# Column-half key sums, a state of own blocks only, and 64-row state products in a linear-attention, gating, Fourier and MLP kernel

## The chip, the cores and the metric

The kernel runs on one core of a Trainium2 chip. The metric is the time of one execution in microseconds (us), as the device measures it; lower is better. The engines are PE (TensorE, matrix products; its weight loads are recorded apart as PEld), DVE (VectorE), ACT (ScalarE), POOL (GpSimd) and SP (here the queue that issues the loads). They run side by side and wait for each other by semaphores.

## The reference, cut to what matters

Three stages run over 4 batch entries of 768 tokens. The first is a linear attention with decay, of 8 heads with 48 features each:

```
for t in range(S):
    state = alpha[:, :, t, :, None] * state + np.einsum('bhd,bhe->bhde', k[:, :, t], v[:, :, t])
    y[:, :, t] = np.einsum('bhd,bhde->bhe', q[:, :, t], state)
```

Its output (384 features a token) goes through a causal depthwise convolution of 5 taps whose sigmoid gates `x @ w_val`, then through `w_out`. The last stage adds the real part of a 2-D Fourier transform, normalises each token, and adds `max(un @ w_ch1, 0) @ w_ch2` with 1536 hidden features.

## The kernel before

**Attention by chunks.** The 768 tokens of a batch entry are taken in 6 chunks (`c` = 0 to 5) of 128. The 8 heads stand in 4 pairs (`p`, `NP` = 4): the even head of a pair (`e` = 0) has its 48 key features on partitions 0 to 47, the odd one (`e` = 1) on 64 to 111. For each chunk:

- `load`, `inv`, `scale` (DVE): scans that form the running decays, then the decayed keys `kd` and queries `qd`.
- `scores`: PE transposes `kd` into the PSUM bank `sums` (L881, 4 transposes) and forms the scores of each head from 48 rows, even heads into the bank `evens`, odd heads into `odds` (L886, 8 matmuls). ACT copies the transposes to `kdT` (L580). Not needed after chunk 5, so there the transposes, the copy and the next two items are left out.
- `sum` (PE, L895): the keys-times-values sum of the chunk, one matmul per pair, 128 stationary columns (both heads' keys) by 112 moving columns of `v_in` (both heads' values). Of the products, those of one head's keys with the other head's values are not needed.
- `state` (DVE, L757 and L761): per head half (64 partitions by 4x48) old state plus new sum, times the decay at the chunk's end. The tile `state` holds 96 columns per pair; the columns of the other head are zero, set once at the start (L703), so that a product over all 128 rows sees one head only.
- `mask` (DVE, L742): both score banks, masked, to `scores`. 
- `y` (PE, `y_of`): output features on partitions, 32 at a time. All outputs go to the bank `evens`, whose blocks 0 and 1 hold the first 32 features (`DA`) of the 8 heads and block 2 the last 16 (`DB`) of each. The part from the state, for c > 0, has 8 matmuls for the first 32 features (L911) and 4 for the last 16 of both heads of a pair (L914), all of 128 rows by 32 stationary columns and 128 moving columns. The part from the scores has 8 (L919) and 8 (L924).
- ACT copies the three blocks to `xT` (L586).

**Order.** Every engine walks the same hand-written list `SCHEDULE`. `prologue()` has the chunks of batch entry 0, with little other PE work among them (`wd` L971, `tapj` L965). `front(b)` has the middle stages of entry b, and for b = 1 and 2 also chunk 0 of the next entry. `mlp(b)` has the MLP of entry b in slots: one `h` (L854, 9 matmuls) and one `down` (L939, 6 matmuls) each; ACT writes `h_hi` (L628) and DVE `h_lo` (L836) between them. The tables `FIRST` and `LATER` put the chunks of entry b + 1 into the slots: `scores` of a chunk two or more slots ahead of its `sum`, `y` and `state`, which stand together. So of the 24 chunks 6 lie in the prologue, 16 in MLP slots (chunk 0 of entry 1, chunks 1 to 5 of entries 1 to 3) and 2 in the fronts. `sum` runs 20 times, the state part of `y` 20 times.

**Waits.** `scores_of` waits for `s_xc` (the bank copied to `xT`) and `s_st` (the state updated, `sums` free); `chunk_sum` for `s_kdc` (`kdT` copied); `y_of` for `s_mask` and `s_st`.

## Time and profile before

| | us |
|---|---|
| median of 3 runs | 596.6 |
| lowest and highest | 596.46, 596.72 |
| the profiled execution | 598.3 |
| its span, first to last instruction | 596.6 |
| PE busy | 581.7 (98%) |
| PE weight loads busy | 553.2 (93%) |
| DVE busy | 393.9 (66%) |
| ACT busy | 198.1 (33%) |

The span of the profiled execution equals the median of the timed runs; 1.7 us of its own 598.3 lie outside the span. In the profile an fp32 matmul appears as two records, so the 4 matmuls of L895 are "x8". Records of PE overlap, so the pace is read from the starts, not from the durations.

### The profile page before, as it was taken

How to read it: one execution, taken by the hardware profiler on the slowest of the kernel's cores; microseconds unless marked ns; L12 is line 12 of the kernel's file. 1: busy time of each engine (PE TensorE's matmuls, PEld its weight loads, DVE VectorE, ACT ScalarE, POOL GpSimd, SP SyncE). 2: the span in 40 equal slices, each digit the busy share in tenths (PEclk: the TensorE clock that was granted, in tenths of full speed). 3: DMA queues.
4: the chain of work that ended last, by engine and by line, in shares of the span. 5: the costliest groups of instructions: out<-in, count | busy, mean ns of one | idle time of the engine just before them, and what ended most of it. 6: DMA issues, size and time to landing. Idle time of an engine off the chain costs nothing.

```text
span 596.6 us, 12364 instructions
## 1 busy us (share of the span) xinstructions
PE 581.7 (98%) x5181; PEld 553.2 (93%) x5181; DVE 393.9 (66%) x835; ACT 198.1 (33%) x437; POOL 14.0 (2%) x31
## 2 busy tenths in 40 slices
PE   7999999999999999999999999999999999999996
PEld 6788999999999999999999999999999999999996
DVE  7579987978948674886947467687855573442221
ACT  5343445424243143324143134222433234222210
POOL 0000000000000000000000000000000000000000
PEclk8999999999999999999999999999999999999999
DMA  7667001232222002033202002033100000000000
GB/s 270 218 220 332 1 18 53 69 113 70 76 73 70 26 3 68 20 120 96 69 11 86 28 2 69 1 89 96 52 1 28 1 27 1 1 2 27 3 25 26
DMA packets 16857, 38.23 MB, mean 64 GB/s; under 512 B 2337, under 2 KB 5410, under 8 KB 16546
## 3 DMA queue, kind: packets, MB, share of 16 engines
q1 hardware_dynamic: 14976, 32.71, 16.5%
q0 software_dynamic: 1536, 4.72, 2.2%
q8 instruction: 41, 0.67, 0.5%
q14 instruction: 14, 0.11, 0.1%
q10 hardware_dynamic: 290, 0.01, 0.0%
HBM read 32.71 MB, written 4.72 MB: 63 GB/s over the span
## 4 chain that ended last, share of the span: by engine, by line
PE 91%; DVE 3%; ACT 2%; issue 2%; DMA 1%; POOL 0%; ACTq 0%; DVEq 0%
PE bank L854 47%; PE bank L939 24%; PE evens L886 4%; PE sums L895 3%; PE bank L965 2%; PE evens L911 2%; PE evens L919 2%; PE evens L924 2%; PE bank L1028 1%; PE bank L1002 1%; PE sums L881 1%; PE bank L971 1%; DVE unT_lo L635 1%; ACT diag L545 1%; PE evens L914 1%
## 5 line engine op out<-in xcount | busy, mean ns | idle before, releaser
L836 DVE SCALAR_TENSOR_TENSOR h_lo<-bank,h_hi 128x256 fp32r<-128x256 f32 x144 | 60.5, 421 | 116.7 <-ACT h_hi L628 113.6
L854 PE MATMUL bank<-unT_hi,w_hi 128*128 128x256 f32 x432 | 125.4, 290 | 2.3 <-DVE unT_lo L635 2.2
L854 PE MATMUL bank<-unT_lo,w_hi 128*128 128x256 f32 x432 | 122.0, 282 | 0.0
L854 PE MATMUL bank<-unT_hi,w_lo 128*128 128x256 f32 x432 | 121.6, 281 | 0.0
L628 ACT ACTIVATE h_hi<-bank 128x256 fp32r<-128x256 f32 x144 | 54.9, 381 | 185.6 <-PE bank L854 185.6
L939 PE MATMUL bank<-w_hi,h_hi 128*128 128x384 f32 x288 | 99.3, 345 | 0.0
L939 PE MATMUL bank<-w_lo,h_hi 128*128 128x384 f32 x288 | 97.7, 339 | 0.0
L939 PE MATMUL bank<-w_hi,h_lo 128*128 128x384 f32 x288 | 97.2, 338 | 0.0
L854 PEld LDWEIGHTS bank<-unT_hi,w_hi 128*128 128x128 f32 x432 | 81.2, 188 | 8.5 <-DVE unT_lo L635 4.5
L854 PEld LDWEIGHTS bank<-unT_hi,w_lo 128*128 128x128 f32 x432 | 81.6, 189 | 0.0
L854 PEld LDWEIGHTS bank<-unT_lo,w_hi 128*128 128x128 f32 x432 | 81.4, 189 | 0.0
L939 PEld LDWEIGHTS bank<-w_hi,h_hi 128*128 128x128 f32 x288 | 54.1, 188 | 2.5 <-issue 2.5
L939 PEld LDWEIGHTS bank<-w_lo,h_hi 128*128 128x128 f32 x288 | 54.1, 188 | 0.0
L939 PEld LDWEIGHTS bank<-w_hi,h_lo 128*128 128x128 f32 x288 | 54.1, 188 | 0.0
L771 DVE SCALAR_TENSOR_TENSOR gate<-xT,wconv,gate 128x384 f32<-128x384 f32 x72 | 42.3, 611 | 0.4
L729 DVE TENSOR_TENSOR_SCAN kd<-a_in,ends 128x516 f32<-128x516 f32 x24 | 29.6, 1233 | 0.8
L720 DVE TENSOR_TENSOR_SCAN lam<-a_in,starts 128x516 f32<-128x516 f32 x24 | 29.4, 1224 | 0.8 <-DMA a_in<-in_alpha_dram 0.8
L586 ACT ACTIVATE xT<-evens 128x384 f32<-128x384 f32 x24 | 11.8, 492 | 49.7 <-PE evens L924 49.7
L886 PE MATMUL odds<-qd,kd 48*128 48x128 f32 x192 | 27.7, 285 | 0.0
L886 PE MATMUL evens<-qd,kd 48*128 48x128 f32 x192 | 27.7, 285 | 0.0
L886 PEld LDWEIGHTS evens<-qd,kd 48*128 48x128 f32 x192 | 23.1, 187 | 4.3 <-issue 4.3
L508 POOL DMA_DIRECT2D out_dram<-u x24 | 13.0, 547 | 576.0 <-DVE u L842 576.0
(159 smaller groups left out, 1102.6 us busy)
## 6 DMA issues: line engine op xcount, KB each, us to landing
a_in<-in_alpha_dram SPq DMA_DIRECT2D x24, 258.5 KB, 2.7
q_in<-in_q_dram SPq DMA_DIRECT2D x24, 256.0 KB, 2.8
k_in<-in_k_dram SPq DMA_DIRECT2D x24, 256.0 KB, 3.2
v_in<-in_v_dram SPq DMA_DIRECT2D x24, 224.0 KB, 3.4
w_raw<-in_w_dram SPq DMA_DIRECT2D x2, 2304.0 KB, 11.5
out_dram<-u POOLq DMA_DIRECT2D x24, 192.0 KB, 2.3
dftd<-in_dft_d_dram SPq DMA_DIRECT2D x1, 582.0 KB, 5.8
woutT<-in_w_out_t_dram SPq DMA_DIRECT2D x1, 576.0 KB, 6.8
```

The lines of the kernel that those rows point to most:

```text
L508: pool.dma_start(out[b, t], u[:, slot(t), :]).then_inc(s_out, 16)
L628: act.activation(h_hi[:, f % HBUF, :], ps[:, 0:GW], ACT.Relu).then_inc(s_hi, 1)
L720: dve.tensor_tensor_scan(lam_[:, :, :].rearrange("d p t -> d (p t)"), a_t[:, 0:NP * CW], starts[:, :, :].rearrange("d p t -> d (p t)"), 0. ...
L729: dve.tensor_tensor_scan(kd_[:, :, :].rearrange("d p t -> d (p t)")[:, ::-1], a_t[:, NP * CW:0:-1], ends[:, NP * CW:0:-1], 0.0, ALU.mult, ...
L771: dve.scalar_tensor_tensor(acc, xT[:, m, t + a * HALF:t + (a + 1) * HALF], wconv[:, m, t:t + 1], acc, ALU.mult, ALU.add).then_inc(s_tap, 1)
L836: dve.scalar_tensor_tensor(h_lo[:, f % HBUF, :], ps[:, 0:GW], 0.0, h_hi[:, f % HBUF, :].bitcast(F32), ALU.max, ALU.subtract).then_inc(s_re ...
L854: last = pe.matmul(ps, l, r, start=(i == 0), stop=(i == len(mms) - 1))
L886: last = pe.matmul(ps[:, p, :], kd_[rows, p, 1:CW], qd_[rows, p, :], start=True, stop=True)
L895: last = pe.matmul(sums[:, p, 0:VW], kdT[:, p, :], v_in[:, c % 2, p, :], start=True, stop=True)
L911: pe.matmul(y[rows, h // 4, :], st[:, h // 2, first:first + DA], qd_[:, h // 2, :], start=(h < 4), stop=False, skip_group_check=True)
L919: pe.matmul(y[rows, h // 4, :], v_[:, h // 2, first:first + DA], scores[:, h % 2, h // 2, :], start=(c == 0 and h < 4), stop=True, skip_gr ...
L939: last = pe.matmul(ps, l[:, f % HBUF, rows], r, start=(f == 0 and x == 0), stop=(f == NF - 1 and x == 2))
```

## The change

- The key sum is 8 matmuls instead of 4: for each pair one per head, 64 stationary columns of `kdT` by that head's 48 columns of `v_in`. The even head's result goes to partitions 0 to 63 of `sums`, the odd head's to 64 to 127, both in columns 0 to 47.
- `state` has 48 columns per pair and no zero blocks, so DVE updates both heads of all pairs in one instruction over 128 partitions, two instructions per chunk instead of four (one instead of two in chunk 0).
- The first 32 features of `y` from the state are 8 matmuls of 64 rows by 32 stationary columns; even heads go to `evens`, odd heads to block 0 of `odds`. The scores part for the first 32 features follows (even heads to `evens`, odd heads to `odds`).
- The last 16 features keep their 128-row products. For these a new tile `tails` holds them with zero blocks. ACT fills it with two copies per chunk (c > 0), placed at `scores`, ahead of the copy to `kdT`; PE waits for the new semaphore `s_tail` between the two groups of state products.
- ACT's copy to `xT` is two instructions, one from each bank. The feature order on the host follows.

```diff
-        state = sb("state", [128, 2, NP, 2 * DH])
+        state = sb("state", [128, 2, NP, DH])
+        tails = sb("tails", [128, 2, NP, 2 * DB])
@@ ACT
-                elif kind == "scores" and a < NCH - 1:
+                elif kind == "scores":
+                    n = b * NCH + a
+                    if a > 0:
+
+                        act.wait_ge(s_st, updates(n - 1))
+                        wait_for(act, s_y, n - 1)
+                        for e, cols in ((0, slice(DA, DH)), (1, slice(0, DB))):
+                            rows = slice(64 * e, 64 * e + 64)
+                            last = act.activation(tails[rows, (a + 1) % 2, :, e * DB:(e + 1) * DB],
+                                                  state[rows, (a + 1) % 2, :, cols], ACT.Copy)
+                        last.then_inc(s_tail, 1)
+                    if a == NCH - 1:
+                        continue
                     act.wait_ge(s_kdT, updates(b * NCH + a))
@@
-                    act.activation(xT[:, :, PAD + a * CH:PAD + (a + 1) * CH], evens[:, 0:K, :],
-                                   ACT.Copy).then_inc(s_xc, 1)
+                    here = slice(PAD + a * CH, PAD + (a + 1) * CH)
+                    act.activation(xT[:, 0:K - 1, here], evens[:, 0:K - 1, :], ACT.Copy)
+                    act.activation(xT[:, K - 1, here], odds[:, 0, :], ACT.Copy).then_inc(s_xc, 1)
@@ DVE
+                    new = sums[:, :, 0:DH]
+                    if c > 0:
+                        dve.tensor_tensor(state_new[:, :, :], new, state[:, (c + 1) % 2], ALU.add).then_inc(s_stn, 1)
+                        dve.wait_ge(s_stn, b * (NCH - 2) + c)
+                        new = state_new[:, :, :]
+                    dve.tensor_tensor(state[:, c % 2], new, fin[:, c % 2, :].unsqueeze(2).broadcast_to([128, NP, DH]),
+                                      ALU.mult).then_inc(s_st, 1)
@@ PE
-                    last = pe.matmul(sums[:, p, 0:VW], kdT[:, p, :], v_in[:, c % 2, p, :], start=True, stop=True)
+                    for e in range(2):
+                        rows = slice(64 * e, 64 * e + 64)
+                        last = pe.matmul(sums[rows, p, 0:DH], kdT[:, p, rows], v_in[:, c % 2, p, e * 64:e * 64 + DH],
+                                         start=True, stop=True)
@@
-                    for h in range(H):
-                        first = h % 2 * (2 * DH - DA)
-                        rows = slice(32 * (h % 4), 32 * (h % 4) + 32)
-                        pe.matmul(y[rows, h // 4, :], st[:, h // 2, first:first + DA], qd_[:, h // 2, :],
-                                  start=(h < 4), stop=False, skip_group_check=True)
                     for p in range(NP):
-                        pe.matmul(y[32 * p:32 * p + 32, 2, :], st[:, p, DA:DA + 2 * DB], qd_[:, p, :],
+                        for e, y in enumerate((evens, odds)):
+                            rows = slice(64 * e, 64 * e + 64)
+                            pe.matmul(y[32 * p:32 * p + 32, 0, :], st[rows, p, e * DB:e * DB + DA], qd_[rows, p, :],
+                                      start=True, stop=False, skip_group_check=True)
+                    pe.wait_ge(s_tail, updates(n - 1))
+                    for p in range(NP):
+                        pe.matmul(evens[32 * p:32 * p + 32, 1, :], tl[:, p, :], qd_[:, p, :],
                                   start=False, stop=False, skip_group_check=True)
```

PE's list, at chunk 1 of batch entry 1 in an MLP slot, before (L854 is `h`, L939 `down`; sizes are stationary by moving columns):

```order
L854 MATMUL bank<-unT_hi,w_lo 128x256
L895 MATMUL sums<-v_in,kdT 128x112 [waits kd_copied,v_loaded_odd]
L895 MATMUL sums<-v_in,kdT 128x112 x3
L911 MATMUL evens<-qd,state 32x128 [waits state_updated,scores_masked]
L911 MATMUL evens<-qd,state 32x128 x7
L914 MATMUL evens<-qd,state 32x128 x4
L919 MATMUL evens<-scores,v_in 32x128 x8
L924 MATMUL evens<-scores,v_in 32x128 x4
L924 MATMUL evens<-scores,v_in 16x128 x4
L939 MATMUL bank<-w_hi,h_hi 128x384 [waits bank_read_vector]
```

The same place after (L861 is `h`, L950 `down`):

```order
L861 MATMUL bank<-unT_hi,w_lo 128x256
L904 MATMUL sums<-v_in,kdT 64x48 [waits kd_copied,v_loaded_odd]
L904 MATMUL sums<-v_in,kdT 64x48 x7
L921 MATMUL evens<-qd,state 32x128 [waits state_updated,scores_masked]
L921 MATMUL odds<-qd,state 32x128
...
L925 MATMUL evens<-qd,tails 32x128 [waits state_tails_copied]
L925 MATMUL evens<-qd,tails 32x128 x3
L930 MATMUL evens<-scores,v_in 32x128 x4
L930 MATMUL odds<-scores,v_in 32x128 x4
L935 MATMUL evens<-scores,v_in 32x128 x4
L935 MATMUL evens<-scores,v_in 16x128 x4
L950 MATMUL bank<-w_hi,h_hi 128x384 [waits bank_read_vector]
```

Nothing moves against `h` and `down`; the sum has twice as many matmuls of narrower shape, the state part as many as before (8 and 4) with the 8 alternating between the banks, and a wait stands ahead of the last 4.

ACT's list in the prologue, around the copy to `kdT` of chunk 2, before:

```order
L553 ACTIVATE wd_hi<-bank 128x388 [waits unit_done]
L559 ACT_TABLE_LOAD
L559 ACTIVATE gate<-bank 128x2x128 [waits unit_done]
L556 ACTIVATE wd_lo<-bank 128x388 [waits unit_done]
L580 ACTIVATE kdT<-sums 128x512 [waits chunk_summed,kd_transposed]
```

And after:

```order
L555 ACTIVATE wd_hi<-bank 128x388 [waits unit_done]
L561 ACT_TABLE_LOAD
L561 ACTIVATE gate<-bank 128x2x128 [waits unit_done]
L558 ACTIVATE wd_lo<-bank 128x388 [waits unit_done]
L587 ACTIVATE tails<-state 64x4x16 [waits y_ready,state_updated]
L587 ACTIVATE tails<-state 64x4x16
L594 ACTIVATE kdT<-sums 128x512 [waits chunk_summed,kd_transposed]
```

The two copies stand ahead of the copy to `kdT` and of all that ACT does later.

## Rows read from the trace of the kernel before

**Rows 1.** The page: busy time and share of the span by engine.
```profile
PE 581.7 (98%) x5181; PEld 553.2 (93%) x5181; DVE 393.9 (66%) x835; ACT 198.1 (33%) x437; POOL 14.0 (2%) x31
```

**Rows 2.** The page: the chain that ended last, share by engine.
```profile
PE 91%; DVE 3%; ACT 2%; issue 2%; DMA 1%; POOL 0%; ACTq 0%; DVEq 0%
```

**Rows 3.** Timeline of PE, chunk 1 of entry 1 (start, length, engine, line, operands, records).
```profile
117.75 0.28 PE L854 MATMUL bank<-unT_hi,w_lo 128*128 128x256 f32 x1
117.87 1.04 PE L895 MATMUL sums<-v_in,kdT 128*128 128x112 f32 x8
118.84 0.64 PE L911 MATMUL evens<-qd,state 128*32 128x128 f32 x16
119.30 0.40 PE L914 MATMUL evens<-qd,state 128*32 128x128 f32 x8
119.52 0.62 PE L919 MATMUL evens<-scores,v_in 128*32 128x128 f32 x16
119.95 0.62 PE L924 MATMUL evens<-scores,v_in 128*32 128x128 f32 x16
120.50 0.44 PE L939 MATMUL bank<-w_hi,h_hi 128*128 128x384 f32 x1
```

**Rows 4.** Timeline of PE, the scores of a chunk between `down` and `h`.
```profile
163.60 0.34 PE L939 MATMUL bank<-w_lo,h_hi 128*128 128x384 f32 x1
163.78 0.34 PE L939 MATMUL bank<-w_hi,h_lo 128*128 128x384 f32 x1
164.05 0.37 PE L886 MATMUL evens<-qd,kd 48*128 48x128 f32 x1
164.05 0.37 PE L886 MATMUL odds<-qd,kd 48*128 48x128 f32 x1
164.26 0.27 PE L886 MATMUL evens<-qd,kd 48*128 48x128 f32 x1
...
164.94 0.27 PE L886 MATMUL odds<-qd,kd 48*128 48x128 f32 x1
165.14 0.39 PE L854 MATMUL bank<-unT_hi,w_hi 128*128 128x256 f32 x1
```

**Rows 5.** Timeline of PE, the sum of chunk 0 in `front(1)`.
```profile
214.62 1.15 PE L895 MATMUL sums<-v_in,kdT 128*128 128x112 f32 x8
215.53 0.34 PE L854 MATMUL bank<-wd_hi,sum_hi 128*128 128x194 f32 x1
```

**Rows 6.** Timeline of PE, chunk 0 of the prologue.
```profile
10.54 2.02 PE L895 MATMUL sums<-v_in,kdT 128*128 128x112 f32 x8 [0.79 <-ACT kdT L580]
12.49 1.08 PE L919 MATMUL evens<-scores,v_in 128*32 128x128 f32 x16
14.14 0.59 PE L971 MATMUL bank<-dftd,woutT 128*128 128x388 f32 x1
```

**Rows 7.** Windows: busy time by engine; the third number from the right is the granted clock.
```profile
10.50:13.60 3.10, 3.06 (x32) 2.81 (x36) 2.94 (x7) 0.00 (x0) 0.00 (x0) 0.50 0.83 321
13.60:14.20 0.60, 0.60 (x17) 0.35 (x9) 0.60 (x2) 0.00 (x0) 0.00 (x0) 0.79 0.00 0
```

**Rows 8.** Timeline of all engines in the prologue, chunks 3 and 4.
```profile
40.04 0.72 DVE L757 TENSOR_TENSOR state_new<-sums,state 64x192 f32<-64x192 f32 x2
40.79 0.72 DVE L761 TENSOR_TENSOR state<-state_new,fin 64x192 f32<-64x192 f32 x2
...
44.55 0.27 PE L886 MATMUL odds<-qd,kd 48*128 48x128 f32 x1
...
45.65 0.69 DVE L742 TENSOR_TENSOR scores<-evens,mask 128x512 f32<-128x512 f32 x1
```

**Rows 9.** Groups by line and form: busy us, mean ns; idle us before, its end.
```profile
L911 PE MATMUL evens<-qd,state 128*32 128x128 f32 x320 | 12.9, 279 | 2.0 <-DVE scores L742 2.0
L628 ACT ACTIVATE h_hi<-bank 128x256 fp32r<-128x256 f32 x144 | 54.9, 381 | 185.6 <-PE bank L854 185.6
L586 ACT ACTIVATE xT<-evens 128x384 f32<-128x384 f32 x24 | 11.8, 492 | 49.7 <-PE evens L924 49.7
```

More of the change, by code:

```diff
@@ L421, in build @@
         s_st = sem("state_updated")
+        s_tail = sem("state_tails_copied")
         s_xc = sem("x_copied")
@@ L702, in _ @@
             dve.memset(mask[:, :], 1.0).then_inc(s_sets, 1)
-            dve.memset(state[:, :, :, :], 0.0).then_inc(s_sets, 1)
+            dve.memset(tails[:, :, :, :], 0.0).then_inc(s_sets, 1)
             dve.memset(xT[:, :, 0:PAD], 0.0).then_inc(s_sets, 1)
@@ L747, in _ @@
                     wait_for(dve, s_y, n)
-                    parts = []
-                    for e in range(2):
-                        rows = slice(64 * e, 64 * e + 64)
-                        mine = slice(e * DH, (e + 1) * DH)
-                        parts.append((state[rows, (c + 1) % 2, :, mine], state[rows, c % 2, :, mine],
-                                      sums[rows, :, e * (VW - DH):e * (VW - DH) + DH], state_new[rows, :, :],
-                                      fin[rows, c % 2, :].unsqueeze(2).broadcast_to([64, NP, DH])))
-                    for old, st, new_ps, new, end in parts:
-                        if c > 0:
-                            dve.tensor_tensor(new, new_ps, old, ALU.add).then_inc(s_stn, 1)
-                    for e, (old, st, new_ps, new, end) in enumerate(parts):
-                        if c > 0:
-                            dve.wait_ge(s_stn, 2 * (b * (NCH - 2) + c - 1) + e + 1)
-                        last = dve.tensor_tensor(st, new if c > 0 else new_ps, end, ALU.mult)
-                    last.then_inc(s_st, 1)
+                    new = sums[:, :, 0:DH]
[5 more added lines that the diff above has]
+                                      ALU.mult).then_inc(s_st, 1)
                 elif kind == "tap":
@@ L901, in y_of @@
                 _, (_, _, qd_) = buffers(b, c)
-                v_, y, st = v_in[:, c % 2], evens, state[:, (c + 1) % 2]
+                v_, st, tl = v_in[:, c % 2], state[:, (c + 1) % 2], tails[:, (c + 1) % 2]
                 if c == NCH - 1:
@@ L907, in y_of @@
                     pe.wait_ge(s_st, updates(n - 1))
-                    for h in range(H):
-                        first = h % 2 * (2 * DH - DA)
-                        rows = slice(32 * (h % 4), 32 * (h % 4) + 32)
-                        pe.matmul(y[rows, h // 4, :], st[:, h // 2, first:first + DA], qd_[:, h // 2, :],
-                                  start=(h < 4), stop=False, skip_group_check=True)
-                    for p in range(NP):
-                        pe.matmul(y[32 * p:32 * p + 32, 2, :], st[:, p, DA:DA + 2 * DB], qd_[:, p, :],
-                                  start=False, stop=False, skip_group_check=True)
-                for h in range(H):
-                    first = h % 2 * (VW - DA)
-                    rows = slice(32 * (h % 4), 32 * (h % 4) + 32)
-                    pe.matmul(y[rows, h // 4, :], v_[:, h // 2, first:first + DA], scores[:, h % 2, h // 2, :],
-                              start=(c == 0 and h < 4), stop=True, skip_group_check=True)
+                    for p in range(NP):
+                        for e, y in enumerate((evens, odds)):
[5 more added lines that the diff above has]
+                        pe.matmul(evens[32 * p:32 * p + 32, 1, :], tl[:, p, :], qd_[:, p, :],
+                                  start=False, stop=False, skip_group_check=True)
+                for e, y in enumerate((evens, odds)):
+                    for p in range(NP):
+                        first = e * (VW - DA)
+                        pe.matmul(y[32 * p:32 * p + 32, 0, :], v_[:, p, first:first + DA], scores[:, e, p, :],
+                                  start=(c == 0), stop=True, skip_group_check=True)
                 for e, part in ((1, slice(DH, DH + 2 * DB)), (0, slice(DA, DH))):
@@ L923, in y_of @@
                         rows = slice(32 * p, 32 * p + part.stop - part.start)
-                        last = pe.matmul(y[rows, 2, :], v_[:, p, part], scores[:, e, p, :],
+                        last = pe.matmul(evens[rows, 1, :], v_[:, p, part], scores[:, e, p, :],
                                          start=False, stop=True, skip_group_check=True)
@@ L1082, in feature_order @@
     heads = np.arange(D).reshape(H, DH)
-    return np.concatenate([heads[:, :DA].reshape(-1), heads[:, DA:].reshape(-1)])
+    return np.concatenate([heads[0::2, :DA].reshape(-1), heads[:, DA:].reshape(-1), heads[1::2, :DA].reshape(-1)])
 def by_rows(w, n):
```

## The prediction

> **What bounds the kernel now.** I read the page first: PE is busy 98% of the span [rows 1], and the chain that ended last is PE for 91%, DVE for 3%, ACT for 2% [rows 2]. So time taken from PE's list is time gained, except where PE waits. It waits little: the one group of the attention that does is the first state products, 2.0 us in all, for DVE's masks in the prologue [rows 9]. Then the timeline of PE around a chunk in an MLP slot, read by starts. Three things stand there.
>
> *Pace.* With 32 stationary columns, four matmuls with different output strips start together: 8 records of the last-16 state products take 0.22 us (119.30 to 119.52), 16 of the scores part 0.43 [rows 3]. That is a round of four records per 0.11 us. With 48 stationary rows the even and the odd head start together too (164.05 twice), and the starts from 164.26 to 164.94, the second pair to the eighth, are again 0.11 us per pair [rows 4]. So strips of columns run side by side, and so do halves of rows, and a round costs 0.11 us. The key sum, 128 full columns, has one record per 0.11 us: 8 records and the change behind them take 0.97 us [rows 3].
>
> *Change of shape.* From a full matmul to a full one there is no gap (117.75 to 117.87, 0.12, L854's own step). Where the shape changes there is one: L939 to L886 takes 0.27 where L939's step is 0.18, the last L886 to L854 0.20 instead of 0.11 [rows 4], L895 to L911 the 0.09 that 0.97 has over 8 x 0.11 [rows 3]. So 0.09 to 0.10 us per change.
>
> *First load.* Behind a change the first weights are not loaded ahead: the first full-width pair of L886 takes 0.21 instead of 0.11 (+0.10) [rows 4], the first round of 32 columns makes four rounds 0.46 instead of 0.43 (+0.03) [rows 3].
>
> The profiled execution's span is 596.6 us, equal to the median of the runs, so a difference worked out on the span is taken from 596.6.
>
> **The key sum.** Before: 0.97 us. After: 8 pairs of matmuls, 16 records in 8 rounds, if the two column halves run side by side as the strips do. A round loads 64 columns instead of 128 and streams 48 instead of 112. No row has such a round. Nearest is L895 itself, 0.11 us for 128 columns loaded and 112 streamed; scaled by the columns loaded a round takes 0.055, by those streamed 0.047. Upper bound: 0.11, as no round in the rows is shorter, whether it loads 128 columns or 32. I take 0.055, since L895 with 112 streamed and L886 with 128 streamed pace alike, which speaks for the load. The sum in an MLP slot now also changes shape at its entry (0.09), has a first load of 64 columns (between 0.03 and 0.10, say 0.05), 8 rounds (0.44) and the change at the end (0.10): 0.68 us, a gain of 0.29. With rounds of 0.11 it is 1.12 us, a loss of 0.15.
>
> In the two fronts the sum stands behind L886, whose change is there anyway, but the L854 behind it now sees a change and a full first load: 0.05 + 0.44 + 0.10 + 0.10 = 0.69 against 0.91 (214.62 to 215.53) [rows 5], a gain of 0.22.
>
> **State products.** Before: 0.46 + 0.22 = 0.68 us for 12 matmuls, 6 rounds [rows 3]. After, the first 8 are 64 x 32 tiles: two row halves by four strips, all different. Each half of that is in the rows, both together are not. If all eight run side by side they need 2 rounds instead of 4. In the rows starts within a round are 0.01 us apart or less, so eight instead of four add some 0.04. Then comes a new change of shape to the 128-row tails: 0.03 + 0.22 + 0.04 + 0.09 + 0.03 + 0.22 = 0.63 us, a gain of 0.05. Ends: with neither stagger nor a change, 0.46 (gain 0.22); with the eight run as two fours, 4 rounds, 0.81 (loss 0.13).
>
> The TensorEngine Tiling page of the Trainium skill (Key Properties) says that changing the tiling mode drains the engine. That speaks against this change, and the 0.09 to 0.10 us of [rows 3, 4] agrees for the shapes they show; 64 to 128 rows at 32 columns is not among them. Without those gaps the forecast would be about 3 us lower.
>
> **Scores part.** Same count, same shapes, same four strips; the odd heads' bank changes. Nothing.
>
> **DVE.** Four instructions of 64 x 192 become two of 128 x 192: before 0.72 + 0.72 us [rows 8]. DVE's time goes by elements per partition (0.36 for 192, 0.69 for 512 [rows 8]), so 0.72 us go per chunk. Between PE's bounds this buys nothing, except at one place: in the prologue between chunks 3 and 4 DVE is the chain. It runs from the update at 40.04 to the mask at 45.65 without a gap, while PE had ended the scores, last started at 44.55 and 0.27 long, by 44.82 [rows 8]. The mask moves to 44.9, just behind that, a gain of 0.72. Next late there is PE, whose scores wait for the same DVE work and move with it.
>
> **ACT.** Two copies replace one of 0.49 us [rows 9]. From 256 to 384 columns costs 0.11 (0.38 to 0.49), so 128 columns cost 0.27, and both 0.65: +0.16 x 24. Two tail copies of 64 elements come to about 0.22 each by the same line: +0.44 x 20. Some 13 us on an engine that stood idle 185.6 us before `h_hi` alone [rows 9]. Queued behind the tails are the copy to `kdT` and then `h_hi`; the sum needs `kdT` two slots later in the MLP. In the prologue it needs it right behind the scores, but there PE then waits for the masks [rows 9], two of 0.68 us, and the shorter sum has half a microsecond more room. The waits of the tails (state and `y` of the chunk before) are ones that PE's own scores pass anyway. Nothing; without that cover, up to 0.44 us at each of 4 prologue chunks.
>
> **The prologue's other parts.** Chunk 0 runs at the lower clock: 0.50, that is 1.2 GHz, from 10.50 to 13.60 [rows 7]. Its sum takes 1.95 us (10.54 to 12.49) and `y` 1.65 [rows 6]. At twice the durations the new sum is 0.10 + 0.88 + 0.19 = 1.2, a gain of 0.75; but the clock rises at about 13.6 to 14.2 [rows 7] whatever PE does, and work that moves ahead of the rise runs at the lower clock: I take 0.45 (0.3 to 0.75). The sums of chunks 1 to 3 end in the shadow of the masks: nothing. The state products of chunks 1, 2, 4 and 5: 4 x 0.05.
>
> **The sum.** MLP chunks 1 to 4 of three entries: 12 x (0.29 + 0.05) = 4.1. Chunk 5, three times: 0.15. Chunk 0 of entry 1: 0.29. The two fronts: 0.44. Prologue: 0.45 + 0.72 + 0.20 = 1.4. Together 6.4 us, and 596.6 - 6.4 = 590.2 us.
>
> **Rivals.**
>
> *A, the eight state products run as two fours.* For it: no row shows more than four records side by side; 16 starts in 0.43 us are 0.027 each, and PE may not start faster. Against it: within a round starts are 0.01 apart. It costs 0.81 instead of 0.63, 0.18 at each of 19 chunks on PE's path (12 + 3 + 4), 3.4 us: 593.6. The sums do not change, as two records in 0.055 us keep that pace.
>
> The page TensorE: Matmul & The Clock Gate of the Trainium skill (Part 1, "Wait — 56ns, not 53.3ns?") says that start-to-start never drops below about 25 ns, however small the matmul. If that held across tiles it would be this rival; the average of [rows 3] agrees with it, the starts within a round (164.05 and 164.05) do not.
>
> *B, a round costs 0.11 us however narrow.* All rounds in the rows cost that. The sums then lose 0.15 instead of gaining 0.29, 0.44 at 13 places, 5.7; the fronts lose 0.44 each more, 0.9; chunk 0 loses its 0.45. Together 7.1: 597.3, no change that can be told. Against it: at 32 columns the stream of 128 explains the 0.11, at L895 the load does.
>
> *C, slower: 64-row tiles exclude the strips beside them.* The even and odd head of a pair run together, as in [rows 4], but pair follows pair: 8 rounds, 0.88 instead of 0.26 us, 0.62 x 19 = 11.8 us: 602.0. It decides against the kernel from where the eight take 0.34 us more than in my sum (6.4 / 19), 5 rounds in place of 2. Against it: L911 shows four strips side by side with full rows, and the two halves write different banks, as in L886.
>
> *D, ACT or the clock.* The tails hold up the prologue, or the longer wait of PE ahead of the masks lets the clock fall once more there, as it stood at 0.50 behind the wait of 0.79 us for `kdT` [rows 6, 7]; 3.1 us at half the clock cost 1.6. The two together give some 592 to 593.
>
> **Chances.** Forecast with its own bounds 0.60, A 0.17, B 0.09, C 0.07, D 0.07. A measurement here tells 0.2% (1.2 us) from no change. Faster by more than that: forecast, A, D, 0.84. Within it: B with what sits beside it, 0.09. Slower: 0.07. The forecast's own low end: rounds of 0.047 (15 x 0.06) and the changes between two narrow shapes free (19 x 0.09 and 12 x 0.08) take 3.6 more, 586.6. High end: A with sums halfway to rounds of 0.07 (0.12 x 13) gives 595.2. Range 586.6 to 595.2; B and C stay outside.
>
> **What the changed profile would show.** In the timeline at a chunk in an MLP slot: from the first record of the sum (16 of them) to the first state product 0.59 us (0.97 before), and 0.21 instead of 0.12 ahead of it; the state part 0.63. Rounds of 0.11 in the sum mean B; the eight state products' 16 records over 0.43 us mean A, over 0.88 C. PE's wait for the masks should be longer than 2.0 us in the prologue and the mask of chunk 4 about 0.7 closer to the update of chunk 3. DVE's busy time should fall by about 13 us (16 x 0.72 + 4 x 0.36), ACT's rise by as much. Wrong would be the whole reading if the wait for the tails appeared as idle time of PE ahead of their products, or if `h` waited for `h_lo` behind ACT's new copies.

## The result and the profile after

The changed kernel takes 590.7 us (median of 4, 590.45 to 591.12), the kernel before 596.7 beside it (median of 4, 596.46 to 599.72): a ratio of 0.989, 95% interval 0.987 to 0.991. That is 5.9 us less; the forecast was 6.4 less, 590.2 us.

In some executions of most kernels here, the profiled one of before among them ([rows 7]; 598.3 us for a span of 596.6, clock 0.995), the records show a stretch of some microseconds early in the program at half the granted clock, and the kernel before then takes 1.3 to 2.7 us longer. So the two profiles differ by 7.6 us in span (596.6 against 589.0), and the kernels by less.

The page of the changed kernel, span, busy time by engine and the chain by engine:

```profile
span 589.0 us, 12731 instructions
...
PE 571.9 (97%) x5341; PEld 538.8 (91%) x5341; DVE 379.0 (64%) x799; ACT 209.0 (35%) x501; POOL 14.0 (2%) x31
...
PE 90%; DVE 4%; issue 2%; ACT 2%; DMA 1%; SPq 1%; POOL 0%; DVEq 0%
```

PE still bounds the kernel ([rows 1, 2]: 98% and 91%). DVE is 14.9 us less busy, ACT 10.9 more, and neither shows it in the time. DMA has 1% of the chain in both, but after it is another transfer, `woutT`, with the queue that issues it (SPq 1%); it is explained below.

The timeline of PE at a chunk in an MLP slot, after (start, length, engine, line, operands, records), to be laid beside [rows 3]:

```profile
114.66 0.28 PE L861 MATMUL bank<-unT_hi,w_lo 128*128 128x256 f32 x1
114.87 0.67 PE L904 MATMUL sums<-v_in,kdT 128*64 128x48 f32 x16
115.47 0.29 PE L921 MATMUL evens<-qd,state 64*32 64x128 f32 x1
...
115.52 0.29 PE L921 MATMUL odds<-qd,state 64*32 64x128 f32 x1
115.61 0.27 PE L921 MATMUL evens<-qd,state 64*32 64x128 f32 x1
...
115.65 0.27 PE L921 MATMUL odds<-qd,state 64*32 64x128 f32 x1
115.85 0.43 PE L925 MATMUL evens<-qd,tails 128*32 128x128 f32 x8
116.09 0.40 PE L930 MATMUL evens<-scores,v_in 128*32 128x128 f32 x8
```

By starts: the sum now takes 0.60 us to the first state product (114.87 to 115.47), where it took 0.97. Ahead of it stand 0.21 us (114.66 to 114.87), where 0.12 stood. The 16 records of the eight state products start in two groups of eight, each group within 0.05 us (115.47 to 115.52, 115.61 to 115.65), the second 0.14 us behind the first. Behind them comes the change of shape to the tails, 0.20 us from the last start (115.65 to 115.85). The state part as a whole takes 0.62 us (115.47 to 116.09), where it took 0.68. So the chunk gains 0.37 - 0.09 + 0.06 = 0.34 us.

Where the gain went over the program can be read by comparing, chunk by chunk, when the scores part of `y` starts (in the prologue's chunk 0, when the product behind it starts). The kernel before is here taken from an execution without a stretch of low clock (`b_again` below, span 594.8 us against 589.0):

```
place                                    forecast   measured
MLP chunks 1 to 4, three entries             4.1        3.57   (11 x 0.30 to 0.35, one 0.00)
MLP chunk 5, three times                     0.15       0.19
chunk 0 of entries 1 to 3                    0.73       0.93   (0.32, 0.31, 0.30)
prologue, chunk 0                            0.45      -0.19
prologue, chunk 4                     0.72 + 0.05       1.01
prologue, chunks 1, 2, 3 and 5               0.15       0.25
sum                                          6.4        5.76
```

The two spans differ by 5.8 us, the medians by 5.9. Three rows need a cause: the MLP chunk that gains nothing, the prologue's chunk 0 and its chunk 4.

**The MLP chunk without a gain** is chunk 3 of entry 1. The timeline of DVE and PE there:

```profile
137.74 1.23 DVE L735 TENSOR_TENSOR_SCAN lam<-a_in,starts 128x516 f32<-128x516 f32 x1
...
138.88 0.67 DVE L757 TENSOR_TENSOR scores<-evens,mask 128x512 f32<-128x512 f32 x1
...
139.19 0.67 PE L904 MATMUL sums<-v_in,kdT 128*64 128x48 f32 x16
...
139.46 0.68 DVE L757 TENSOR_TENSOR scores<-odds,mask 128x512 f32<-128x512 f32 x1
...
140.20 0.29 PE L921 MATMUL evens<-qd,state 64*32 64x128 f32 x1 [0.34 <-DVE scores L757]
```

The masks stand behind the scan for the next chunk on DVE and end at about 140.1. The long sum of before hid that but for 0.07 us: from its start to the first state product it is 1.04 us there, 0.97 elsewhere.

```profile
142.86 1.04 PE L895 MATMUL sums<-v_in,kdT 128*128 128x112 f32 x8
143.90 0.64 PE L911 MATMUL evens<-qd,state 128*32 128x128 f32 x16
```

The short one ends in front of the masks: 1.01 us from its start to the first state product (139.19 to 140.20), where it is 0.60 elsewhere. That is 0.41 us late where it was 0.07, and the 0.34 between them is all that such a chunk gains.

**Prologue, chunk 0.** The sum ends earlier (11.11), and then a transfer is late:

```profile
10.37 0.67 PE L904 MATMUL sums<-v_in,kdT 128*64 128x48 f32 x16 [0.72 <-ACT kdT L594]
11.11 0.43 PE L930 MATMUL evens<-scores,v_in 128*32 128x128 f32 x8
...
11.57 0.62 PE L935 MATMUL evens<-scores,v_in 128*32 128x128 f32 x16
12.57 0.59 PE L982 MATMUL bank<-dftd,woutT 128*128 128x388 f32 x1 [0.38 <-DMA woutT<-in_w_out_t_dram]
```

From the chain that ended last: `woutT`, issued at 5.15, lands 7.38 us later, at 12.53.

```profile
5.15 7.38 DMA woutT<-in_w_out_t_dram
```

The kernel before, at the same clock, starts that product at 12.38 (shown below). What the sum gives there, the transfer takes in this execution. That is a matter of the execution, though: in the kept traces of the runs below the transfer lands 6.8 to 7.8 us after its issue, and with the short sum, the loads issued in the same order and the clock at 1.00 the product starts at 12.03 (`t_first`), 12.26 (`s_emajor`), 12.57 (here), 12.61 (`p_fill`) or 12.85 (`p_split`). So chunk 0 gives between 0.35 and -0.47 us against the 12.38.

**Prologue, chunk 4.** The timeline of DVE, to be laid beside [rows 8], and PE's first state product:

```profile
38.38 0.33 DVE L765 TENSOR_TENSOR state_new<-sums,state 128x192 f32<-128x192 f32 x1
38.74 0.36 DVE L768 TENSOR_TENSOR state<-state_new,fin 128x192 f32<-128x192 f32 x1
...
43.00 0.67 DVE L757 TENSOR_TENSOR scores<-evens,mask 128x512 f32<-128x512 f32 x1
...
44.32 0.29 PE L921 MATMUL evens<-qd,state 64*32 64x128 f32 x1 [0.79 <-DVE scores L757]
```

From the update to the mask it is 4.62 us (38.38 to 43.00), where it was 5.61 (40.04 to 45.65): 0.99 less. Of this 0.86 lie in the update itself, which takes 0.64 us to the next instruction (38.38 to 39.02) where it took 1.50, and 0.12 between the scan and the mask behind it (1.14 us from start to start, 1.26 before).

### The profile page after: what moved, and what is told of

The parts are those of the page before. It is cut to its first block, busy times and chain, and to the rows that moved or that the text cites. A ratio compares the mean times of both kernels' runs of the same rounds, so it can differ in the third digit from the quotient of the medians.

```text
span 589.0 us, 12731 instructions
## 1 busy us (share of the span) xinstructions
PE 571.9 (97%) x5341; PEld 538.8 (91%) x5341; DVE 379.0 (64%) x799; ACT 209.0 (35%) x501; POOL 14.0 (2%) x31
## 4 chain that ended last, share of the span: by engine, by line
PE 90%; DVE 4%; issue 2%; ACT 2%; DMA 1%; SPq 1%; POOL 0%; DVEq 0%
PE bank L861 47%; PE bank L950 24%; PE evens L893 4%; PE bank L976 2%; PE evens L935 2%; PE sums L904 1%; PE bank L1039 1%; PE bank L1013 1%; PE sums L888 1%; DMA woutT<-in_w_out_t_dram 1%; PE evens L925 1%; PE bank L982 1%; PE evens L921 1%; PE evens L930 1%; PE odds L930 1%
## 5 line engine op out<-in xcount | busy, mean ns | idle before, releaser
L861 PE MATMUL bank<-unT_hi,w_hi 128*128 128x256 f32 x432 | 125.5, 291 | 2.3 <-DVE unT_lo L650 2.2
L861 PE MATMUL bank<-unT_lo,w_hi 128*128 128x256 f32 x432 | 122.2, 283 | 0.0
L861 PE MATMUL bank<-unT_hi,w_lo 128*128 128x256 f32 x432 | 121.8, 282 | 0.0
L950 PE MATMUL bank<-w_hi,h_hi 128*128 128x384 f32 x288 | 99.5, 345 | 0.0
L950 PE MATMUL bank<-w_lo,h_hi 128*128 128x384 f32 x288 | 97.7, 339 | 0.0
L950 PE MATMUL bank<-w_hi,h_lo 128*128 128x384 f32 x288 | 97.3, 338 | 0.0
L861 PEld LDWEIGHTS bank<-unT_hi,w_hi 128*128 128x128 f32 x432 | 81.3, 188 | 8.4 <-DVE unT_lo L650 4.5
L861 PEld LDWEIGHTS bank<-unT_hi,w_lo 128*128 128x128 f32 x432 | 81.8, 189 | 0.0
L861 PEld LDWEIGHTS bank<-unT_lo,w_hi 128*128 128x128 f32 x432 | 81.6, 189 | 0.0
L950 PEld LDWEIGHTS bank<-w_hi,h_hi 128*128 128x128 f32 x288 | 54.2, 188 | 2.5 <-issue 2.5
L950 PEld LDWEIGHTS bank<-w_lo,h_hi 128*128 128x128 f32 x288 | 54.2, 188 | 0.0
L950 PEld LDWEIGHTS bank<-w_hi,h_lo 128*128 128x128 f32 x288 | 54.1, 188 | 0.0
L757 DVE TENSOR_TENSOR scores<-evens,mask 128x512 f32<-128x512 f32 x24 | 16.4, 683 | 14.5 <-PE odds L893 14.5
```

The source lines that it names most:

```text
L757: dve.tensor_tensor(scores[:, e, :, :], ps_, mask[:, :].unsqueeze(1).broadcast_to([128, NP, CH]), ALU.mult).then_inc(s_mask, 1)
L861: last = pe.matmul(ps, l, r, start=(i == 0), stop=(i == len(mms) - 1))
L950: last = pe.matmul(ps, l[:, f % HBUF, rows], r, start=(f == 0 and x == 0), stop=(f == NF - 1 and x == 2))
```

## The experiments

Ratios are against the kernel before, run beside each set. Its median was 596.8 us beside `b_again`, `p_sum`, `p_y` and `p_split`, 596.8 beside `k48`, `s_emajor`, `t_first` and `t_twice`, 596.7 beside `p_fill`, `s_mv32` and `best`, and 598.1 beside `best_busy`.

**The kernel before, unchanged (`b_again`).** Is the stretch of low clock in [rows 7] part of the typical time?

> The kernel before, unchanged. The span of the changed kernel's profile is 7.6 us shorter, its timed median 5.9 us. Theory: the profiled execution of the kernel before was one in which the granted clock fell to 0.50 ahead of chunk 0's sum (mean clock 0.995, 598.3 us), and most executions are without that stretch. Then the runs here split into some near 596.6 us with a mean clock of 0.997 or more and a span near 594.9, and some near 598.3 with 0.995; in one of the first kind the sum of chunk 0 takes about 1.0 us instead of 1.95. Rival: all executions of it have the low stretch, clock 0.995 in each, and the change removed it; then 1.5 us of the gain are the clock's.

Measured: 596.83 us, ratio 1.000 (0.999 to 1.002). Seven of ten executions took 596.5 to 597.1 us at a clock of 0.998 or more, three 598.1 to 599.3 at 0.995 or less. In the profiled one (span 594.8) the stretch is absent, in the timeline of PE and in the window that spans it (third number from the right: granted clock):

```profile
10.32 1.11 PE L895 MATMUL sums<-v_in,kdT 128*128 128x112 f32 x8 [0.68 <-ACT kdT L580]
11.37 0.64 PE L919 MATMUL evens<-scores,v_in 128*32 128x128 f32 x16
...
12.38 0.59 PE L971 MATMUL bank<-dftd,woutT 128*128 128x388 f32 x1
```

```profile
8.00:14.00 6.00, 5.32 (x65) 4.11 (x66) 5.08 (x9) 2.77 (x10) 0.00 (x0) 1.00 0.96 362
```

The sum of chunk 0 takes 1.05 us here, not the 1.95 of [rows 6]. So the term of 0.45 us for chunk 0 was drawn from a state that most executions do not have.

**The key sum alone (`p_sum`).** The kernel before, with one edit (and L753 reading `sums[rows, :, 0:DH]`):

```diff
-   last = pe.matmul(sums[:, p, 0:VW], kdT[:, p, :], v_in[:, c % 2, p, :], start=True, stop=True)
+   for e in range(2):
+       rows = slice(64 * e, 64 * e + 64)
+       last = pe.matmul(sums[rows, p, 0:DH], kdT[:, p, rows], v_in[:, c % 2, p, e * 64:e * 64 + DH], ...)
```

> The kernel before with the key sum alone in column halves (DVE reads columns 0 to 47 of both halves, four instructions as before; state, y and ACT as before). Theory: each sum in an MLP slot ends 0.28 us earlier (0.97 to 0.60, less 0.09 at its entry), 13 of them less the one at chunk 3 of entry 1 that waits for a mask, and 0.29 in each of two fronts: 3.9 us, 592.7 us. Rival: the gain of the whole comes from less work on DVE; then this is within 1 us of the kernel before.

Measured: 593.48 us (592.43, 592.67, 594.29, 594.30), ratio 0.9945 (0.993 to 0.996). The MLP chunks gain 0.25 to 0.28 us each, the fronts 0.29, chunk 3 of entry 1 nothing. The two executions at a clock of 0.999 (592.43, 592.67) agree with what was expected; the other two, at 0.996, are 1.7 us slower, and the profile of one of them has a new stretch of low clock, of which more at `p_split`. DVE's work is unchanged here, so the rival falls.

**The state products, tails and ACT's copies alone (`p_y`)**, with the old sum and four DVE instructions.

> The kernel before with the y part alone: own blocks only in the state, 64-row products into both banks, tails copied by ACT, two copies to xT; the sum is 4 full matmuls and DVE has four instructions per chunk. Theory: 0.055 us a chunk, 15 in MLP slots and 4 or 5 in the prologue: 1.0 us, 595.6. Rival: ACT's 13 us more hold something up, and this is slower than the kernel before, 597 or more.

Measured: 595.88 us, ratio 0.9987 (0.997 to 1.0005); seven of ten took 595.6 to 596.1. Each chunk with state products in an MLP slot gains 0.05 to 0.06 us, but for chunk 3 of entry 1, which stands behind its masks and gains nothing. The interval holds no change; that the gain of some 0.9 us is real is read from the chunks and from those seven executions.

**DVE's part undone (`p_split`)**: the changed kernel with four instructions of 64 x 192 in place of two of 128 x 192.

> The changed kernel with DVE's update in four instructions of 64 rows instead of two of 128. Theory: DVE's part is worth only what it gives between chunks 3 and 4 of the prologue, 0.7 to 1.0 us: 591.6. Rival: DVE's relief works in the MLP too (it goes into waits of PE for h_lo and unT_lo): 593 or more.

Measured: 592.99 us (591.74 to 593.80), ratio 0.993 (0.991 to 0.995), so 2.3 us above the changed kernel, near the rival's number. But the MLP chunks stand within 0.05 us of the changed kernel's, so the rival's reason does not hold: the loss is in the prologue. The profile shows two parts there. The timeline of PE at the prologue's chunk 4, and the windows ahead of it and behind it:

```profile
43.34 0.67 PE L911 MATMUL sums<-v_in,kdT 128*64 128x48 f32 x16
45.59 0.29 PE L928 MATMUL evens<-qd,state 64*32 64x128 f32 x1 [1.58 <-DVE scores L757]
```

```profile
42.00:45.70 3.70, 2.12 (x43) 1.71 (x49) 3.60 (x7) 2.33 (x5) 0.00 (x0) 1.00 1.02 433
45.80:49.20 3.40, 3.40 (x60) 2.66 (x45) 3.29 (x7) 0.55 (x2) 0.00 (x0) 0.53 0.99 417
```

PE waits 1.58 us for the mask (0.79 in the changed kernel), and the granted clock then stands at 0.53, the lower level (1.2 GHz) for nearly all of 3.4 us. The other part is what DVE's four instructions cost by themselves: the quickest execution is 591.74, 1.3 us above the quickest of the changed kernel. `p_sum` shows the same picture, a wait of 1.57 us and then 0.53. In the kernel before (trace of `b_again`) PE waits 1.10 us there, and the clock stays at 1.00:

```profile
45.23 0.64 PE L911 MATMUL evens<-qd,state 128*32 128x128 f32 x16 [1.10 <-DVE scores L742]
```

```profile
45.20:48.70 3.50, 3.47 (x72) 3.25 (x73) 3.36 (x8) 0.49 (x1) 0.00 (x0) 1.00 1.02 434
```

**Is it the idle time? (`p_fill`)** `p_split`, with the sum of that one chunk formed three times over, so that PE is busy while DVE masks:

```diff
-   for p in range(NP):
+   for p in [p for _ in range(3 if (b, c) == (0, 4) else 1) for p in range(NP)]:
```

> The changed kernel with DVE's update in four instructions (593.0 us, with a stretch of granted clock 0.50 from 45.8 us), and the sum of prologue chunk 4 done three times over, so that PE, which waited 1.6 us for the masks there, waits 0.7 us. Same results, and the added matmuls lie in the wait. Theory: the longer idle of PE lets the clock fall; with it filled the stretch is gone and the time is 591.6 in every undisturbed execution. Rival: the stretches of lower clock come by chance, whatever PE does there: 592 to 593 with runs on both sides as before.

Measured: 592.09 us (591.74 to 592.31), ratio 0.991 (0.989 to 0.993). By the medians the added work made the kernel 0.9 us quicker, and the spread fell from 2.1 to 0.6 us. The intervals of the two ratios overlap, so it is the profile that settles it:

```profile
43.11 1.60 PE L911 MATMUL sums<-v_in,kdT 128*64 128x48 f32 x48
45.36 0.29 PE L928 MATMUL evens<-qd,state 64*32 64x128 f32 x1 [0.64 <-DVE scores L757]
```

```profile
45.80:49.20 3.40, 3.40 (x62) 3.19 (x60) 3.29 (x7) 0.55 (x2) 0.00 (x0) 1.00 1.01 428
```

The clock stays at 1.00 in the same window, and all four executions had a clock of 0.997 or more, against one of four in `p_split`. Idle PE ahead of that place opens the way to the lower clock there; it does not force it, since two of `p_sum`'s four executions, with the same list, had a clock of 0.999. What decides between executions is not shown. What is left against the changed kernel, 1.4 us by the medians, stands in the trace at two places: 1.00 us at chunk 4, which is DVE's share, and 0.31 at chunk 5, which was not taken apart.

The page TensorE: Matmul & The Clock Gate of the Trainium skill (Part 1, "What's actually happening") says that the clock is set by how busy the engine has been; this pair agrees.

**What sets the pace of the narrow rounds?** Three kernels change the sum of the changed kernel. `k48` loads 48 stationary columns in place of 64:

```diff
-   last = pe.matmul(sums[rows, p, 0:DH], kdT[:, p, rows], ...)
+   last = pe.matmul(sums[64*e:64*e+DH, p, 0:DH], kdT[:, p, 64*e:64*e+DH], ...)
```

> The changed kernel with 48 instead of 64 stationary columns in each half of the key sum (the 16 left out are padding). In the changed kernel a round of the sum (even and odd head side by side) took 0.058 us. Theory: the load of 64 columns sets it, so 48 columns give 0.044 to 0.048, 8 rounds 0.08 to 0.11 us less, at 15 sums outside the prologue 1.2 to 1.6 us: 589.3. Rival: starts set it (two records in 0.058 us), or the stream of 48: rounds stay at 0.058, 590.7.

`s_mv32` streams 32 moving columns in place of 48:

> The changed kernel with 32 instead of 48 moving columns in each half of the sum (64 stationary as in the changed kernel); a third of the value features is left out of the sums. Theory: the load of 64 stationary columns sets the round, which stays at 0.058 us. Rival: the stream sets it: 0.042 or less, and 8 rounds take 0.13 us less.

`s_emajor` forms the even heads of all four pairs first and then the odd ones, so that neighbours in the list share one column half:

> The changed kernel with the sum's 8 matmuls in another order: the even heads of the four pairs first, then the odd ones, instead of even and odd in turn. Theory: matmuls run in the order written, so four in a row in one column half have nothing beside them and the sum takes nearly twice as long, 16 steps of 0.05 to 0.06 us, +0.4 us at 13 places: 596. Rival: PE looks ahead past the matmuls of the one half, and the time stays at 590.7.

Timelines of PE from the sum to the first state product, of `k48`, of `s_mv32` and of `s_emajor`:

```profile
115.53 0.56 PE L903 MATMUL sums<-v_in,kdT 128*48 128x48 f32 x16
116.03 0.29 PE L920 MATMUL evens<-qd,state 64*32 64x128 f32 x1
```

```profile
115.71 0.66 PE L904 MATMUL sums<-v_in,kdT 128*64 128x32 f32 x16
116.30 0.29 PE L921 MATMUL evens<-qd,state 64*32 64x128 f32 x1
```

```profile
115.00 0.94 PE L904 MATMUL sums<-v_in,kdT 128*64 128x48 f32 x16
115.87 0.29 PE L921 MATMUL evens<-qd,state 64*32 64x128 f32 x1
```

0.50, 0.59 and 0.87 us, against 0.60 in the changed kernel. The sum is a first round of 0.08 to 0.09 us, six more and a last one with the change behind it. A third less to stream changes nothing measurable in the pace of the rounds (0.058 us in both). A quarter less to load takes 0.10 us from the eight of them: read from record to record a round is 0.045 us in `k48` (its last begins 0.35 us into the sum, at 115.88; in the changed kernel 0.44, at 115.31). That is the 0.044 to 0.048 of the theory. The load sets the pace. And the order matters: with the halves grouped, the odd half starts 0.27 us into the sum and only part of the two overlaps. Times: `k48` 589.1 us, 1.6 below the changed kernel, ratio 0.986 (0.984 to 0.989), the two executions at a clock of 0.999 588.9 and 589.05; `s_emajor` 594.5, ratio 0.996 (0.995 to 0.998), between what both theories gave it; `s_mv32` 591.4 in its one execution, with a stretch of low clock (mean 0.995), so its time says nothing and its timeline is what counts.

**The price of a change of shape (`t_first`).** The tails' products are moved ahead of the 64-row ones, which puts one change more into the list (to 32 columns, to 64 rows, back to 128 rows):

```diff
+   pe.wait_ge(s_tail, updates(n - 1))
+   for p in range(NP):
+       pe.matmul(evens[32 * p:32 * p + 32, 1, :], tl[:, p, :], qd_[:, p, :], start=True, ...)
    for p in range(NP):
        for e, y in enumerate((evens, odds)):
...
-           pe.matmul(y[32 * p:32 * p + 32, 0, :], st[rows, ...], qd_[rows, p, :], start=True, ...)
+           pe.matmul(y[32 * p:32 * p + 32, 0, :], st[rows, ...], qd_[rows, p, :], start=(e == 1), ...)
-   pe.wait_ge(s_tail, updates(n - 1))
-   for p in range(NP):
-       pe.matmul(evens[32 * p:32 * p + 32, 1, :], tl[:, p, :], qd_[:, p, :], start=False, ...)
```

> The changed kernel with the 128-row products of the tails ahead of the 64-row state products instead of behind them. Same matmuls, one more change of shape per chunk (128 to 64 rows and back to 128). Theory: the price of a change is 0.09 plus 0.03 for the first load, so 0.12 us at 19 chunks, 2.3 us: 593.0. Rival: with 32 columns on both sides the gap is not a price of the row shape (in the changed kernel's trace 0.20 from the last start to the first tail could be the wait for the tails' semaphore), and the time stays at 590.7.

Measured: 593.18 us, ratio 0.994 (0.993 to 0.996), 2.45 us above the changed kernel, or 0.13 at each of 19 chunks. Its timeline of PE:

```profile
115.47 0.43 PE L920 MATMUL evens<-qd,tails 128*32 128x128 f32 x8
115.83 0.29 PE L925 MATMUL evens<-qd,state 64*32 64x128 f32 x1
...
116.01 0.27 PE L925 MATMUL odds<-qd,state 64*32 64x128 f32 x1
116.21 0.43 PE L930 MATMUL evens<-scores,v_in 128*32 128x128 f32 x8
```

0.74 us for the same products (115.47 to 116.21), where the other order takes 0.62. The rival falls: the 0.20 us from the last state product to what follows stands here too (116.01 to 116.21), ahead of the scores part, which waits for no tails. The page TensorEngine Tiling of the Trainium skill (Key Properties) says that a change of mode drains the engine; this is its price here, first load included.

**ACT's tail copies doubled (`t_twice`)**, the second copies into a tile that nobody reads.

> The changed kernel with ACT's tail copies doubled (two more to a spare tile, 0.5 us at each of 20 chunks, ahead of the copy to kdT). Theory: ACT's copies are covered: in MLP slots the sum comes two slots later, in the prologue PE waits for the masks; 590.7 to 591.2. Rival: ACT's added work is what keeps the gain small, and another 10 us of it cost 2 us or more: 593.

Measured: 592.66 us (590.38, 591.90, 593.41, 594.44), ratio 0.991 (0.988 to 0.994). The median is the rival's number, but not for the rival's reason. The MLP chunks stand within 0.05 us of the changed kernel's, and the execution with a clock of 0.998 took 590.38, no more than the changed kernel. So the copies themselves are hidden. The other three show clocks of 0.990 to 0.995. In the profiled one the lower clock (window, and ACT's timeline) lies ahead of the first tail copy:

```profile
4.40:18.00 13.60, 11.12 (x87) 7.92 (x86) 9.57 (x14) 6.23 (x22) 0.00 (x0) 0.63 0.82 306
```

```profile
19.96 0.24 ACT L588 ACTIVATE tails<-state 64x64 f32<-64x64 f32 x1
```

So there at least the copies did not bring it; the other two executions have no trace.

**A version that takes what was left (`best`).** `k48`, with the two places of above mended: the scans of chunk 4 one step later in the list of DVE's work, which puts the masks of chunk 3 ahead of them, and the loads of `dftd` and `woutT` issued ahead of the `v` of chunk 1:

```diff
-         "load": (None, 3, 7, 10, 14, 18, 26), "inv": (None, 4, 8, 11, 15, 19, 28),
+         "load": (None, 3, 7, 10, 15, 18, 26), "inv": (None, 4, 8, 11, 16, 19, 28),
...
+                if n == 1:
+                    sp.dma_start(dftd[:, :, :], dft_d).then_inc(s_dload, 16)
+                    sp.dma_start(woutT[:, :, :], w_out_t).then_inc(s_dload, 16)
                 wait_for(sp, s_y, n - 1)
                 sp.dma_start(v_in[:, c % 2], v[b, c]).then_inc(s_v[c % 2], 16)
```

> The changed kernel with 48 stationary columns in the sum, and two places mended at which its trace shows a gain lost: the loads for the first Fourier product (dft matrix, transposed w_out) are issued ahead of chunk 1's values, since that product started only when the second of them had landed at 12.53 us; and in the slots of entry 0's MLP the decay scans of chunk 4 stand one slot later, behind the masks of chunk 3, for which PE waited 0.41 us. Theory: 589.1 less 0.3 to 0.4 at the mask and up to 0.35 at chunk 0: 588.5. Rival: both stalls only move on (to the scores of chunk 4, to the queue of the first loads), and it stays at 589.1.

Measured: 589.26 us (588.33, 588.42, 588.60, 589.92, 591.23, 592.65), ratio 0.987 (0.985 to 0.990). Its timeline of PE at the two places:

```profile
12.13 0.59 PE L980 MATMUL bank<-dftd,woutT 128*128 128x388 f32 x1
```

```profile
138.46 0.56 PE L902 MATMUL sums<-v_in,kdT 128*48 128x48 f32 x16
138.95 0.29 PE L919 MATMUL evens<-qd,state 64*32 64x128 f32 x1
```

Chunk 3 of entry 1 gains 0.52 us on the changed kernel (0.49 from the sum's start to the first state product, where it was 1.01): 0.41 of wait and 0.10 of the narrower load. That mend is shown. At chunk 0 the product starts 0.44 us sooner than in the changed kernel's trace, without a wait, but `t_first` has it at 12.03 with the loads in their old order, so how much of this the new order gives is not shown; the masks hold PE up by 0.18 us there now. The three executions at a clock of 0.998 or more took 588.3 to 588.6 us, those of `k48` 588.9 and 589.05. Three of six had low clocks (0.989 to 0.994), and by the medians the two kernels cannot be told apart; by those at a high clock it is some 0.5 us, with three executions against two.

**Can the early stretch be filled away too? (`best_busy`)** `best`, with five products of the identity while ACT copies `kdT` of chunk 0, the sums of the prologue's chunks 1 to 3 formed twice and that of chunk 4 three times.

> The kernel of the run best with work for PE in its waits of the prologue: 5 matmuls of the identity while chunk 0's kdT is copied, and the sums of chunks 1 to 3 done twice and of chunk 4 three times (same results). Of best's six executions three had a mean clock of 0.994 or less and took 589.9 to 592.7, the others 588.3 to 588.6. Theory: idle PE in the prologue is what lets the clock fall; with it filled all executions lie near 588.4 with a mean clock of 0.997 or more. Rival: the stretches early in the program come from elsewhere (they are seen in the kernel before too), and again a third or more of the executions take 590 or longer.

Measured: 589.44 us (588.64 to 591.98), ratio 0.986 (0.984 to 0.988) to a kernel before that had low clocks in most of its executions this time (median 598.1). Three of six are still at 590 or above, two of them at clocks of 0.995 and 0.993; the third, 590.04, is at 0.999, and what it lost is not known. Filled waits did not keep the lower clock out, so the idle time that was filled is not the only cause; whether it is one, two of six against three of six in `best` do not tell. What brings the early stretch in some executions and not in others stays open.

## Why the prediction was right, and where not

The bound (PE's list), the sign and the size held: 5.9 us where 6.4 were forecast, and the terms that make up most of it, the sums and the state products in MLP slots, are right in their mechanism too. That the total comes so near is in part luck: chunk 0 of the prologue (0.6) and the MLP chunks (0.5) gave less than forecast, chunk 4 of the prologue, the fronts and the small chunks 0.6 more. By its steps:

- *The key sum.* 0.68 us with its entry was forecast, a gain of 0.29. The sum took 0.60 + 0.09 = 0.69, and `p_sum` gained 0.27 to 0.28. A round takes 0.058 us (0.055 forecast), with 48 columns loaded 0.045, and `k48` and `s_mv32` show that the reason given, the load, is the right one. Rival B falls.
- *The fronts.* 0.22 us each was forecast, 0.30 measured. The mis-sized term is the second 0.10, the full first load of the L854 behind the sum: the kernel before already had that load exposed, 0.17 us from the first to the second start there (215.53 to 215.70), against 0.19 after. To the first start it is 0.91 against 0.61.
- *State products.* A gain of 0.05 was forecast, 0.06 measured, 0.63 against 0.62 us. Eight tiles start together, stagger 0.05 us (the end of 0.46 without it and without a change is 0.47 by its own terms); rivals A and C fall with the same rows. Rival A's other ground goes too. The page TensorE: Matmul & The Clock Gate of the Trainium skill (Part 1, "Wait — 56ns, not 53.3ns?") has a start-to-start floor of about 25 ns; across tiles it does not hold here, where eight starts lie 6 to 7 ns apart. For one tile no run comes near it.
- *Changes of shape.* 0.09 for the drain and 0.03 for a first load were forecast; `t_first` puts the two together at 0.13 us.
- *Twelve MLP chunks.* Eleven gained. The step that failed is "It waits little", read from a sum over the program (and the first state products are not the only group of the attention that waits: L895 waits 0.79 us [rows 6]). A wait that hardly showed, because the long sum covered all but 0.07 us of it, took the gain of chunk 3 of entry 1. Worth 0.34 us; the rest of the 0.5 is that the eleven gained 0.33 on the mean, not 0.34, and the forecast's rounding.
- *Prologue, chunk 0.* 0.45 forecast, -0.19 measured between the two traces. Two faults: the term was taken at a clock that the median execution does not have, and the load of `woutT` was left out of account. In the trace of before it lands at 11.8 (issued at 5.03, 6.8 us), over 2 us ahead of the product at 14.14; only at the full clock, with the product due at 12.1 to 12.4, is it the next late thing. Worth 0.6 us, the largest miss, with 0.8 us of play from execution to execution. That the clock rises "whatever PE does" no run shows; in `b_again`'s trace it does not fall there at all.
- *The starting point.* That the profiled span equals the median was taken for agreement. In truth 1.7 to 1.8 us lie outside the span in every execution (590.8 against 589.0, 596.53 against 594.8), and the profiled one of before was 1.7 us slow. The two cancelled.
- *Prologue, chunk 4.* 0.72 forecast for DVE's instructions, 0.99 gained between update and mask. Of the 0.27 more, 0.14 lies in the update itself (1.50 to 0.64 us, where the durations gave 0.72), and 0.12 ahead of the mask, its cause open. The forecast took the scores of PE to be just ahead of the mask; they moved along, as it said.
- *ACT, and rival D.* The copies are hidden (`t_twice`), ACT has 10.9 us more where 13 were forecast, DVE 14.9 less where 13 were: `p_split`'s page has 392.8 us, so 13.8 are the update's, and the memset of zeros shrank from 0.70 to 0.27. PE's wait for the masks rose from 2.0 to 2.6 us, as forecast. The clock half of D exists, though not in the changed kernel's trace: those of `p_sum` and `p_split` have it behind 1.57 and 1.58 us of idle PE, the changed kernel's, with 0.79, does not. DVE's part, forecast for its 0.72 us, also keeps that idle time short.

## What to carry to other kernels

Where PE is the bound and a product computes blocks that nobody reads, splitting it into tiles that run side by side pays by the columns loaded per round, if neighbours in the list alternate between the tiles and no change of shape (0.13 us here) is added for each saving. Before booking such a gain at every place, look at each for the next late thing, a mask or a transfer, that the long product had covered; here one chunk gave nothing, and at another the gain hung on when a transfer landed. And take the granted clock of the profiled execution beside that of the timed ones before a row at half the clock goes into a sum.

## What was not expected of the hardware

- Eight 64-row by 32-column tiles run at once: 16 records in two groups of eight, each started within 0.05 us, on two PSUM banks.
- The columns loaded per tile decide the pace of a round even where they are few, as long as no more are streamed: 128 loaded 0.11 us, 64 loaded 0.058, 48 loaded 0.045.
- The order of issue limits the overlap: the same 16 records take 0.60 us with the halves alternating and 0.87 grouped.
- Added products made a kernel 0.9 us quicker by the medians of four executions each (`p_fill`); its trace has the granted clock at 1.00 where it had been 0.53 for 3.4 us.
